# Attention scores on four quarters of the array

## What is computed

```python
batch, n_heads, seq, head_dim = (4, 8, 768, 48)
f = 1.0 / (1.0 + np.exp(-f_logit))
state = np.zeros((B, H, D, D))
for t in range(S):
    state = f[:, :, t, :, None] * state + np.einsum('bhd,bhe->bhde', k[:, :, t], v[:, :, t])
    y[:, :, t] = np.einsum('bhd,bhde->bhe', q[:, :, t], state)
```

## Time and profile before

| what | value |
|---|---|
| runs | 1230.0, 1232.95, 1232.96 us; median 1232.95 |
| profiled execution | span 1221.6 us from the first to the last instruction |
| outside the span (median less span) | 11.3 us |
| PE busy | 1185.8 us, 97% |
| DVE busy | 687.1 us, 56% |
| ACT busy | 481.6 us, 39% |
| POOL busy | 479.4 us, 39% |
| score matmuls (L1850) | start at 12.9 us, last at 283.9 us |

### The profile page before, as it was taken

The page is one execution under the profiler, slowest core; times in us unless marked ns, Lnnn a source line. Parts: engine busy times, 40 slices in busy tenths (PEclk is TensorE's granted clock), DMA queues, the critical chain, the costliest instruction groups (busy, mean ns, idle before and its releaser), DMA issues.

```text
span 1221.6 us, 25186 instructions
## 1 busy us (share of the span) xinstructions
PE 1185.8 (97%) x8085; PEld 1037.9 (85%) x8086; DVE 687.1 (56%) x1215; ACT 481.6 (39%) x968; POOL 479.4 (39%) x463
## 2 busy tenths in 40 slices
PE   4999999999999999999999999999999999999998
PEld 4777787788888999999999998888888888888887
DVE  7888988887534454544444554445445454454433
ACT  4666665556333343433333443332322323223212
POOL 8458777754573617163357552220020200100000
PEclk9999999999999999999999999999999999999999
DMA  6233343343577868687788864130030301201000
GB/s 229 72 112 122 123 140 101 109 167 124 188 234 236 250 199 260 202 255 224 237 248 267 248 221 145 52 104 27 28 77 26 104 27 45 60 26 52 27 1 26
DMA packets 109523, 164.78 MB, mean 135 GB/s; under 512 B 48384, under 2 KB 85504, under 8 KB 108928
## 3 DMA queue, kind: packets, MB, share of 16 engines
q1 hardware_dynamic: 97584, 115.48, 30.5%
q0 software_dynamic: 11712, 47.98, 12.6%
q10 hardware_dynamic: 144, 0.20, 0.0%
HBM read 107.45 MB, written 56.16 MB: 134 GB/s over the span
## 4 chain that ended last, share of the span: by engine, by line
PE 82%; POOL 6%; DVE 4%; issue 3%; ACT 2%; DMA 2%; SPq 0%; DVEq 0%; POOLq 0%; ACTq 0%
PE pD L2041 17%; PE pD L2152 12%; PE pA L2152 12%; PE pA L2073 9%; PE pS L2073 9%; PE pA L2180 6%; PE pA L1850 5%; PE pX L2180 3%; PE pS L2180 3%; DVE W L1315 1%; POOL qk L728 1%; POOL fT L709 1%; POOL prods L744 1%; DMA stage<-w 1%; POOL qk L727 1%
## 5 line engine op out<-in xcount | busy, mean ns | idle before, releaser
L2041 PE MATMUL pD<-we,xsH 128*128 x612 | 189.6, 391 | 0.1
L1850 PE MATMUL pA<-W 64*128 64x128 f32 (+3 forms) x1920 | 136.8, 283 | 15.7 <-DVE W L1315 12.2
L1763 DVE TENSOR_TENSOR gs<-pD,sig 128x512 f32<-128x512 f32 x71 | 49.1, 692 | 169.3 <-ACT sig L1229 169.3
L1850 PEld LDWEIGHTS pA<-W 64*128 64x128 f32 (+3 forms) x1920 | 112.7, 170 | 34.8 <-DVE W L1315 18.7
L948 POOL DMA_INDIRECT pair<-y_sorted,y_row x40 | 38.8, 970 | 248.9 <-DMA z_rows<-pair 229.5
L2041 PEld LDWEIGHTS pD<-we,xsH 128*128 128x128 f32 x612 | 114.1, 188 | 22.2 <-issue 0.5
L2041 PE MATMUL pD<-we,xsL 128*128 x306 | 120.1, 392 | 0.0
L1229 ACT ACTIVATE sig<-pD 128x512 f32<-128x512 f32 x71 | 42.6, 600 | 192.4 <-PE pA L2152 192.4
L1315 DVE TENSOR_TENSOR W<-W,prods 128x512 f32<-128x512 f32 (+1 forms) x120 | 101.9, 856 | 22.9 <-PE pA L1850 20.8
L2073 PE MATMUL pA<-we,hidH 128*128 (+1 forms) x448 | 114.5, 336 | 0.0
L1495 DVE STREAM_TRANSPOSE pA<-hidP 128x512 f32<-128x512 f32 x98 | 64.6, 705 | 81.5 <-DMA hidP<-hid_rows 81.3
(11 more groups left out here) (315 smaller groups left out, 2660.9 us busy)
## 6 DMA issues: line engine op xcount, KB each, us to landing
hid_rows<-hid SPq DMA_DIRECT2D x49, 512.0 KB, 3.4
hidP<-hid_rows SPq DMA_DIRECT2D x196, 128.0 KB, 2.9
stage<-w POOLq DMA_DIRECT2D x48, 384.0 KB, 4.7
qk<-qk_t SPq DMA_DIRECT2D x24, 512.0 KB, 3.7
y_sorted<-yo SPq DMA_DIRECT2D x53, 192.0 KB
xs<-x_sorted SPq DMA_DIRECT2D x200, 48.0 KB, 2.1
fT<-f_t SPq DMA_DIRECT2D x12, 512.0 KB, 4.2
vN<-v_n SPq DMA_DIRECT2D x24, 256.0 KB, 2.7
```

The source lines that it names most:

```text
L1763: dve.tensor_tensor(gs[:], pD[:, f % 2 * 512:f % 2 * 512 + TT], sig[f % 2][:], ALU.mult).then_inc(s_u, 1)
L1850: ins = pe.matmul(pA[par][keys, s, c * P:(c + 1) * P], both[r, 1, c, keys], both[r, 0, c], start=True, stop=True)
L2041: ins = pe.matmul(hidden_bank(t, h), (xsL if a else xsH)[t.par][:, k * P:(k + 1) * P], we[:, bass.ds(at + (b * WE + k * F + h * HF), HF)], ...
```

## The change

In `scores`, the 128 keys and 128 queries are no longer multiplied whole. Half-blocks of 64 keys meet 64 queries: for fills 0 to 4 the left keys meet the left queries and the right keys the right queries, in two matmuls in place of one; for fill 5 the left keys meet the right queries, in one. The four products that go to (left, right) keys and (upper, lower) row halves use four different quarters of the array. Fill 0 of the tiles 0 and 1 stays whole, since `pA` holds nothing yet. The limit on keys at fills 3 to 5 (112, 96 and 64 keys) is gone; the parts that are left out of the product are read by no one, or are masked. `LEVELS`, the order of work and all waits stay.

```diff
--- before.py
+++ after.py
@@ -1843,12 +1843,18 @@
                     else:
                         pe.wait_ge(s_rect[par], RECTS * i + n - MASKED)
                 both = W[t % 6] if n else qk[t % 4]
+                left, right, whole = slice(0, HS), slice(HS, P), slice(0, P)
+                blocks = ((left, left), (right, right))
+                if n == 0 and t < 2:
+                    blocks = ((whole, whole),)
+                if n == NL:
+                    blocks = ((left, right),)
                 for c in range(HP):
-                    for s in range(2):
-                        r = slice(HS * s, HS * (s + 1))
-                        keys = slice(0, P - LEVELS[n - 1] if n >= MASKED else P)
-                        ins = pe.matmul(pA[par][keys, s, c * P:(c + 1) * P], both[r, 1, c, keys], both[r, 0, c],
-                                        start=True, stop=True)
+                    for keys, asks in blocks:
+                        for s in range(2):
+                            r = slice(HS * s, HS * (s + 1))
+                            ins = pe.matmul(pA[par][keys, s, c * P:(c + 1) * P][:, asks], both[r, 1, c, keys],
+                                            both[r, 0, c, asks], start=True, stop=True)
                 ins.then_inc(s_a[par], 1)
 
             def turn_keys(t):
```

## The result

The change takes 1234.35 us (median of 13 runs, 1230.0 to 1238.68), the kernel before 1230.87 us on the same chip (13 runs, 1228.96 to 1232.96). The ratio is 1.0027, interval 1.0016 to 1.0039: slower by a little, where I forecast 15.5 us less. Device times in this document are medians of fast executions; one execution of the kernel with the top level alone, 1301.94 us at a clock of 0.853, was slow and is left out.

What follows compares the result with a forecast made beforehand. PE was taken as first bound, DVE second. Attention savings of 9.8 + 3.0 + 1.4 + 1.3 = 15.5 us took the 1221.6 us span to 1206.1, plus 11.3 outside it: 1217.5 us, range 1209 to 1230.

Steps and rivals of the forecast that it cites:

- The fill: 0.63 us: Score fills on PE: all four array quarters go together, so a fill falls from 1.09 us to 0.63 us.
- The rival that the quarters take turns: Score fills: quarters of one row half alternate, 1.08 us a fill below the top; 1228.5 us in all; chance 0.15.
- that of no overlap: Score fills: neither stream nor load overlaps within a row half, 1.96 us a fill; about 1317 us; chance 0.06.
- The path's share: Attention: of 5.3 us PE saving a pair, the path keeps 1.3 us, 3.9 us in three pairs.
- POOL's chain: Second pair: the chain through POOL to `stateD` is late next; `stateD` comes 2.75 us earlier, DVE's wait there lasts.
- the saving is carried to the end: After the attention: PE is full and released by work ending with the attention, so all 15.5 us reach the end.
- PE's gaps in the attention would be well under that: Clock rival, attention: PE gaps stay well under 2.14 us; at worst one half-clock stretch, 1.7 us; no chance given.
- They cost what the steps above count: PE: some 1900 more matmul records and as many loads cost nothing beyond the steps counted in a fill.
- all terms but the 1.3 behind it: Attention savings 9.8, 3.0 and 1.4 us, without 1.3 us from three fills after the weight transfer.
- 11.3 us lie outside the span: Whole run: median 1232.95 us against profiled span 1221.6 us; the 11.3 us between were left unchanged.
- the cap of 14.3 + 6.2 us: Attention, eight pairs: DVE's idle time caps the gain from faster PE at 20.5 us, 2.6 us a pair.

Runs made afterwards that it cites:

- the kernel with the top level alone: Kernel before with only the top-level fill cut to left keys by right queries, other levels whole: 1225.57 us, ratio 0.9993.
- the filled change: The change plus throwaway matmuls before top fills, one for the even tile, two for the odd: 1215.74 us, 0.9926; 1.0092 on another chip.
- the left half alone: The change without right keys by right queries below the top level: 1227.63 us, 1.0018 of the kernel before; again 1228.58 us, 1.0019.
- the filled changes: The change with throwaway matmuls before top fills, one or two for the second tile: 1215.45 us (0.9921) and 1215.74 us (0.9926).
- the product at level 4: The change with one and two throwaway matmuls before top fills, plus one of 256 columns at level 4, odd tile: 1239.45 us, 1.0059; elsewhere 1.0074.
- The kernel before with fillers: Kernel before, whole fills, plus throwaway matmuls before top fills, one for the even tile and two for the odd: 1246.65 us, 1.0127.
- The kernel with wide queries: The change, but each half-block of 64 keys meets all 128 queries: 1225.43 us, 0.9996 of the kernel before; again 1225.2 us, 0.9995.
- the first two levels alone: Kernel before with levels 0, 1 and the top in quarters, levels 2 to 4 whole: 1221.14 us, 0.9958; on another chip 1.0056.

## Why the prediction was wrong

**What held.** The fill: 0.63 us, with all four quarters going together. The rival that the quarters take turns is out, and so is that of no overlap. The rule of the Trainium skill that spoke against it (TensorE: Matmul & The Clock Gate, What overlaps and what doesn't: a weight load overlaps only matmuls of another row group) doesn't hold here: 32 loads, half of them next to a matmul of their own row group, fit into 0.63 us with their matmuls. The path's share can come out: 3.9 us in three pairs was forecast, and 69.01 - 65.11 = 3.9 us was measured in one stretch of the filled change's quickest execution, where the clock stayed up and nothing stalled, 2.6 in the next. POOL's chain behaved as forecast (waits for `stateD` stay), and the saving is carried to the end: that execution's first expert matmul is at 276.16, 13.4 us before that of the kernel before, and its span 12.3 us shorter. By the medians the filled change is 9.5 to 9.8 us faster on that chip, not 15.5.

**What failed, first: the clock.** "PE's gaps in the attention would be well under that; at worst one such stretch, 1.7 us, is inside my range." I took one row, a fall after 2.14 us of idle, for a bound, and compared only the length of single gaps with it. With the change PE's waits for DVE grew to 26.5 us in 23 (up to 2.0 us), and the granted clock fell nearly every time that one pair gave way to the next (the router's logits there take 1.08 us instead of 0.64 in nine of eleven cases). The falls shown came within a wait of 1.43 us behind one of 0.57, and in one experiment within a wait of 0.81 us behind two of 0.58 and 1.43. About 58 us of the attention ran at 1.2 GHz, where I allowed one stretch of 3.5. It hits the worst place, the chain of PE between two pairs: 6.26 us, where the filled change takes 3.71 for the same work. The Trainium skill has this too (TensorE: Matmul & The Clock Gate, A second HAM failure mode: psum-queue depth-cycling: frequent small idles between groups of matmuls let the clock fall and rise all the time), and the trace agrees: 23 waits in 184 us, with a mean clock of 0.87.

That the clock falls, and that work on the chain between pairs then takes longer, is shown. How much of the result it explains is not. On the quick chips the left half alone, low clock without stalls, begins the last pair at 258.68; the filled changes begin it at 251.14 (the quickest execution, clock 0.99) and at 257.02 (clock 0.95). The price is thus 7.5 us or 1.7, with the fillers' own time on the other side. There the fillers go with a gain of 0.7 to 0.8%, but the change without them is missing beside them. On the two slower chips, where a filled kernel and the change ran side by side, the fillers raised the clock and took no time off (medians 2.9 us higher, with the product at level 4, and 3.9 us). So the clock alone doesn't explain the loss on the kind of chip that gave the result.

**Second: the price of more records.** "They cost what the steps above count" of 1900 more matmul records and as many loads. On the quick chips this held for the filled change. On the others, that of the result among them, PE stops inside dense stretches of short fills, and the signals of finished fills come late. The prediction has no term for this. The change begins its last pair at 269.16 us, the left half alone at 258.68: 10.5 us, in part also the lower clock that stalls lengthen, and in part what else differs between the two chips. In three pairs the two late signals seen in the result's trace (2.36 and 1.55 us) are 3.9 us, and the period is 71.65 - 68.27 = 3.4 us longer than that of the left half alone. The same filled change begins its last pair at 251.14 on one chip and at 273.46 on another. The kernel before with fillers has no stall on a chip where the change stalls, and the change with fillers none on a quick chip, apart from a gap of 1.2 us: it takes both the short fills and such a chip.

Together: the forecast for the last pair is 263.96 less 14.2 (all terms but the 1.3 behind it), 249.8; from there it is 1.3 us to the filled change's quickest execution, 7.5 more to the left half alone, and 10.5 more to the change, 269.1. These are differences of consecutive positions, so they must add up; they come from single executions on three chips. With the filled change's other trace the first two would be 7.2 and 1.7.

**A third, smaller:** "11.3 us lie outside the span". Only 1.6 us do (device time 1231.14 us, span 1229.5). The execution profiled before was thus one of some 1223.3 us, and quicker than all the runs listed with it: it fits the chips on which the kernel before takes 1225 us. My stretches and waits were read from a quick chip, and the time was added up for another. With 1.6 us the same saving would have given 1207.7 us for a quick chip; the filled changes came to 1215.45 and 1215.74 there. That these lie near my 1217.5 is luck. One more number can't be followed from the rows: the cap of 14.3 + 6.2 us has 13.4 us of the earlier trace rows and 0.9 us that DVE's mask copies waited for fills. Nothing in the forecast hangs on it.

**Open.** What the stalls are isn't known. That PE waits for its instructions to be fetched was my theory, and two things speak against its plainest form. In the result's trace no packet of the instruction queue that grew from 53 to 68 falls into 119.7 to 129.5 us or 173.8 to 177.5 us, around the stalls that end at 127.09 and 175.66. And 15 more packets for 3776 more records of matmuls and loads are some 250 records a packet; moving the program by 128 records, half of that, didn't move the stalls. The kernel with wide queries, as many instructions at a slower pace, met only quick chips, so many long instructions on a slower chip are untested. Nor is it known what sets the chips apart. The change itself, without fillers, wasn't run on a quick chip; by the left half alone I would expect up to 0.4% less time there.

**The better version.** The change with fillers, or the first two levels alone, beats the kernel before on some chips (0.9921 and 0.9926, 0.9958) and loses on others (1.0092, 1.0056). None that I ran is better than the kernel before on all.

## What to carry to other kernels

When a change takes work off TensorE in a stretch where it alternates with another engine, look at what it then waits for and where: idle time ahead of a chain that others wait for can bring the lower clock just there, and make that chain longer than it was. Add up such waits; one row with the length of a single gap is no bound. A throwaway matmul in the gap tests it, but only beside the new kernel without it, and the old one, on the same chip. Splitting matmuls into quarters pays only if the records can be issued that fast, and one chip's trace doesn't settle this: run such a kernel on several.

## What the runs showed of the hardware

- Four 64 x 64 quarters of the array work together: 32 fp32 records with 64 moving columns in 0.63 us, 20 ns from one to the next on average, the first four within 0.03 us.
- The granted clock fell within a wait of 1.43 us (0.57 us of waiting shortly before it), and in one kernel within a wait of 0.81 us (0.58 and 1.43 us before it); the kernel before kept 1.00 over a wait of 1.44 us. The same work took 3.71 us at the upper clock and 6.26 us with the lower one.
- From 84 to 268 us a kernel with 88% busy PE kept a clock of 0.99, one with 91% had 0.94.
- Chips differ: the kernel before took 1225 to 1226 us on some, 1231 to 1232 us on others, and the same edited kernel 0.9926 and 1.0092 of it. On the latter PE made gaps of 0.4 us within a fill, and VectorE waited up to 3.3 us for the signals of fills; the kernel before with fillers, whole fills alone, showed neither on such a chip.
